# Attention in two-part float32 on one core: raw queries loaded once, their low part written to the other half, masks in three operations

## The reference

```python
scores = scale * np.matmul(q, k.transpose(0, 1, 3, 2))
rel = pos[:, None] - pos[None, :]
is_global = pos[None, :] < int(n_global)
is_local = (rel >= 0) & (rel < int(n_local))
keep = is_global | is_local
dist = np.where(is_global & ~is_local, float(n_local), np.abs(rel).astype(np.float32))
bias = -slopes[:, None, None] * dist[None, :, :]
scores = np.where(keep, scores + bias, -1000000000.0)
a = softmax(scores); out = a @ v
```

## Time and profile before

| what | value |
|---|---|
| median of 3 runs | 793.82 us (793.75 to 794.51) |
| profiled execution | 794.11 us; its span 792.4 us |
| busy time in the span | PE 740.9 us (94%), DVE 548.1 (69%), ACT 461.7 (58%), POOL 165.9 (21%) |
| attention | from the start to about 220 us |
| DMA | 151.65 MB, mean 191 GB/s |
| raw loads in attention | k_raw 64 x 208 KB, q_raw 64 x 192 KB |

### The profile page before, as it was taken

One profiled execution on the slowest core, in us unless ns is written; L12 is line 12 of the kernel. 1 busy time (PEld: TensorE's weight loads), 2 busy tenths in 40 slices (PEclk: granted clock), 3 DMA queues, 4 the chain that ended last, 5 costly groups with the idle time before them and its releaser, 6 DMA issues. The chain is left out here.

```text
span 792.4 us, 15792 instructions
## 1 busy us (share of the span) xinstructions
PE 740.9 (94%) x5585; PEld 662.7 (84%) x5588; DVE 548.1 (69%) x1499; ACT 461.7 (58%) x931; POOL 165.9 (21%) x189
## 2 busy tenths in 40 slices
PE   2899999999959999999999839999999999999997
PEld 2799999999938888898888627888888888889895
DVE  6878778777477979887777667767675758585420
ACT  3889899899535555565545315454636363636360
POOL 8100000000030232222321202142323232323221
PEclk9999999999969999999999959999999999999999
DMA  8999988986264676545763126676767676759751
GB/s 178 218 212 247 242 213 232 203 233 155 98 211 156 223 248 229 188 143 196 252 232 113 36 77 210 187 222 186 222 185 220 186 223 186 221 169 314 230 120 43
DMA packets 64106, 151.65 MB, mean 191 GB/s; under 512 B 12294, under 2 KB 15750, under 8 KB 64016
## 3 DMA queue, kind: packets, MB, share of 16 engines
q1 hardware_dynamic: 52512, 114.77, 49.2%
q0 software_dynamic: 11504, 35.72, 18.0%
HBM read 118.84 MB, written 16.67 MB: 171 GB/s over the span
## 5 line engine op out<-in xcount | busy, mean ns | idle before, releaser
L2006 PE MATMUL r_ph<-r_xh,r_w1h 128*128 128x384 f32 x256 | 90.7, 354 | 0.0
L2006 PE MATMUL r_ph<-r_xh,r_w1l 128*128 128x384 f32 x256 | 86.2, 337 | 0.0
L2006 PE MATMUL r_ph<-r_xl,r_w1h 128*128 128x384 f32 x256 | 85.8, 335 | 0.0
L604 ACT ACTIVATE pr<-pr,nmx 128x232 f32<-128x232 f32 (+1 forms) x192 | 79.9, 466 | 4.3 <-DVE nmx L710 2.9
L710 DVE CUSTOM_DVE_ANT_0 pr<-sc,bias 128x232 f32<-128x232 f32 (+1 forms) x192 | 65.0, 375 | 19.0 <-PE sc L478 17.7
L611 ACT ACTIVATE prt<-tp 128x384 f32<-128x384 f32 (+1 forms) x128 | 65.4, 536 | 20.4 <-PE tp L490 16.9
L2020 PE MATMUL r_py<-r_w2h,r_hh 128*128 128x512 f32 x192 | 76.3, 398 | 0.0
L2020 PE MATMUL r_py<-r_w2h,r_hl 128*128 128x512 f32 x192 | 75.1, 391 | 0.0
L2020 PE MATMUL r_py<-r_w2l,r_hh 128*128 128x512 f32 x192 | 74.9, 390 | 0.0
L518 PE MATMUL op<-vo,prt 128*128 128x128 f32 x384 | 69.5, 276 | 3.7 <-ACT prt L611 1.9
L477 PE MATMUL sc<-kk,qh 128*128 128x256 f32 x192 | 59.0, 328 | 14.7 <-POOL alive L439 14.3
(11 more groups left out here) (340 smaller groups left out, 1970.4 us busy)
## 6 DMA issues: line engine op xcount, KB each, us to landing
r_w<-moe_w SPq DMA_DIRECT2D x64, 512.0 KB, 5.7
m_w<-moe_w SPq DMA_DIRECT2D x36, 512.0 KB, 6.3
row_buf<-moe_w SPq DMA_DIRECT2D x9, 2048.0 KB, 8.4
r_w2l<-r_w POOLq DMA_DIRECT2D x32, 512.0 KB, 5.4
k_raw<-kI SPq DMA_DIRECT2D x64, 208.0 KB, 6.8
q_raw<-qT SPq DMA_DIRECT2D x64, 192.0 KB, 7.3
vo<-vL SPq DMA_DIRECT2D x16, 384.0 KB
x_rows<-row_buf SPq DMA_DIRECT2D x4, 1536.0 KB, 6.2
```

Of the source, the lines that this page charges most:

```text
L604: nc.scalar.activation(pr[n % PRS][:, t, lo:CW], pr[n % PRS][:, t, lo:CW], ACT.Exp, bias=nmx[n % PRS][:, t:t + 1], scale=-1.0).then_inc(ex ...
L2006: last = nc.tensor.matmul(ph[m % 4][:, 0:CAP], w[:, c, m * P:(m + 1) * P], x[:, c, :], start=(c == 0 and a == 0), stop=(c == KC - 1 and a ...
```

## The change

Raw queries are loaded once per head, into partitions 0 to 63; k is still loaded twice. `qq` holds q's high part in its upper half and q's low part in its lower half: DVE reads partitions 0 to 63 and writes 64 to 127. `kh` is k's high part in both halves, `kl` k's low part in partitions 0 to 63. The first product is qq with kh over 128 rows (high with high, low with high), the second qq's high half with kl over 64 rows. The zero memsets go.

The limits are loaded from ACT's queue, ahead of its first activation; SP starts with the raw loads, in the order pair 0, v of pair 0, pair 1, v of pair 1. POOL writes 768 into `rel` for keys after the query (one more link). DVE scales `rel` by 2^-40 before the limits arrive; masks are then three operations of full size (distances in units of 2^-40, capped by the limit for global keys, and whole numbers for masked keys), and a head's bias is one product per table. The third split now follows the first maxima, the fourth the second; the bias tables of heads 1 to 7 stand in steps 2, 5, 8, ... 20; the splits of pair 1 move by one step.

```diff
-def mask(link, rel, kpos, lims, isg, loc, keep, dist, shift=0.0, between=None):
+def mask(link, rel, kpos, lims, isg, loc, keep, dist, shift=0.0):
...
-            qh = [fb(f"qh{s}", [P, 2, S], F32R) for s in range(2)]
-            ql = [fb(f"ql{s}", [P, 2, S], F32R) for s in range(2)]
-            kk = [fb(f"kk{s}", [P, 2, KW], F32R) for s in range(2)]
+            qq = [fb(f"qq{s}", [P, 2, S], F32R) for s in range(2)]
+            kh = [fb(f"kh{s}", [P, 2, KW], F32R) for s in range(2)]
+            kl = [fb(f"kl{s}", [P, 2, KW], F32R) for s in range(2)]
...
                     for half in range(2):
-                        w = slice(half * D, half * D + D)
-                        sp.dma_start(k_raw[s][w, hh, :], kI[g, hh]).then_inc(raw_loaded[s][hh], 16)
-                        sp.dma_start(q_raw[s][w, hh, :], qT[g, hh * D:hh * D + D]).then_inc(raw_loaded[s][hh], 16)
+                        sp.dma_start(k_raw[s][half * D:half * D + D, hh, :], kI[g, hh]).then_inc(raw_loaded[s][hh], 16)
+                    sp.dma_start(q_raw[s][0:D, hh, :], qT[g, hh * D:hh * D + D]).then_inc(raw_loaded[s][hh], 16)
...
-                sp.dma_start(ints[:, 0:1], n_global.partition_broadcast(P)).then_inc(ints_loaded, 16)
-                sp.dma_start(ints[:, 1:2], n_local.partition_broadcast(P)).then_inc(ints_loaded, 16)
                 load_raw(0)
-                load_head(1, 0)
                 load_v(0)
-                load_head(1, 1)
+                load_raw(1)
                 load_v(1)
...
+                link(g.affine_select(out=rel[:, CA:].rearrange("p (t j) -> p t j", j=P), in_=rel[:, CA:].rearrange("p (t j) -> p t j", j=P),
+                                     compare_op=ALU.is_ge, fill=float(S), base=0, pattern=[[0, 2], [-1, P]], channel_multiplier=1))
                 assert link.n == RELS
-                link(g.memset(ql[0][D:P].bitcast(F32), 0.0))
...
-                link(g.memset(ql[1][D:P].bitcast(F32), 0.0))
...
-                        nc.tensor.matmul(to, qh[s][:, hh, q], kk[s][:, hh, keys], start=True, stop=False)
-                        last = nc.tensor.matmul(to, ql[s][:, hh, q], kk[s][:, hh, keys], start=False, stop=True)
+                        nc.tensor.matmul(to, qq[s][:, hh, q], kh[s][:, hh, keys], start=True, stop=False)
+                        last = nc.tensor.matmul(to, qq[s][0:D, hh, q], kl[s][0:D, hh, keys], start=False, stop=True)
...
-                    dst, src = (kk[s][:, hh, :], k_raw[s][:, hh, :]) if is_k else (qh[s][:, hh, :], q_raw[s][:, hh, :])
+                    dst, src = (kh[s][:, hh, :], k_raw[s][:, hh, :]) if is_k else (qq[s][0:D, hh, :], q_raw[s][0:D, hh, :])
...
+                act.dma_start(ints[:, 0:1], n_global.partition_broadcast(P)).then_inc(ints_loaded, 16)
+                act.dma_start(ints[:, 1:2], n_local.partition_broadcast(P)).then_inc(ints_loaded, 16)
                 act.wait_ge(filled, 1)
...
-                        g, c = n // 6 + 1, n % 6 - 1
+                        g, c = n // 6 + 1, n % 6 - (2 if n < 6 else 1)
...
-                dve.wait_ge(ints_loaded, 2 * 16)
                 dve.wait_ge(filled, RELS)
+                link(v.tensor_scalar(rel_units[:], rel[:], UNIT, None, ALU.mult))
+                dve.wait_ge(ints_loaded, 2 * 16)
...
-                        w = slice(D, P)
-                        ins = v.tensor_tensor(kk[s][w, hh, :], k_raw[s][w, hh, :], kk[s][w, hh, :].bitcast(F32), ALU.subtract)
+                        ins = v.tensor_tensor(kl[s][0:D, hh, :], k_raw[s][0:D, hh, :], kh[s][0:D, hh, :].bitcast(F32), ALU.subtract)
                     else:
-                        ins = v.tensor_tensor(ql[s][0:D, hh, :], q_raw[s][0:D, hh, :], qh[s][0:D, hh, :].bitcast(F32), ALU.subtract)
+                        ins = v.tensor_tensor(qq[s][D:P, hh, :], q_raw[s][0:D, hh, :], qq[s][0:D, hh, :].bitcast(F32), ALU.subtract)
...
-                        v.scalar_tensor_tensor(out=dst[:, h, :], in0=dist[:, w], scalar=-slope, in1=pen[:, w],
-                                               op0=ALU.mult, op1=ALU.add).then_inc(biased, 1)
+                        v.tensor_scalar(dst[:, h, :], dist[:, w], -slope / UNIT, None, ALU.mult).then_inc(biased, 1)
...
-                    mask(link, rel[:], kpos[:], lims, isg[:], loc[:], tmp[:], dist[:], between=first_parts)
-                    link(v.tensor_scalar(pen[:], tmp[:], 1.0, BIG, ALU.subtract, ALU.mult))
+                    link(v.tensor_scalar(local_units[:], lims[:, 1:2], UNIT, None, ALU.mult))
+                    link(v.tensor_scalar(outside[:], kpos[:], lims[:, 0:1], None, ALU.is_ge))
+                    link(v.scalar_tensor_tensor(out=far[:], in0=rel[:], scalar=lims[:, 1:2], in1=rel_units[:], op0=ALU.is_ge, op1=ALU.max))
+                    for c in (0, 1):
+                        split(0, c)
+                    link(v.scalar_tensor_tensor(out=dist[:], in0=outside[:], scalar=local_units[:], in1=far[:], op0=ALU.max, op1=ALU.min))
                     biases(0)
-                    dve.wait_ge(biased, 3)
-                    split(0, 2)
                     for n in range(STEPS):
                         if n < ALL_UNITS:
                             maxima(n)
-                        if n == 0:
-                            split(0, 3)
-                        if 1 <= n < H:
-                            biases(n)
+                        if n < 2:
+                            split(0, 2 + n)
+                        if n % 3 == 2 and n // 3 + 1 < H:
+                            biases(n // 3 + 1)
...
-                        g, c = n // 6 + 1, n % 6 - 2
+                        g, c = n // 6 + 1, n % 6 - (3 if n < 6 else 2)
                         if g < PAIRS and 0 <= c < PARTS:
                             split(g, c)
+                        elif n == 6:
+                            split(1, PARTS - 1)
```

More of the change, by code:

```diff
@@ L41 @@
 BIG = 8e9
+UNIT = 2.0 ** -40
 SCALE = D ** -0.5
@@ L102, in mask @@
     link(v.scalar_tensor_tensor(out=loc, in0=dist, scalar=lims[:, 1:2], in1=keep, op0=ALU.is_lt, op1=ALU.mult))
-    if between is not None:
-        between()
     link(v.tensor_tensor(dist, loc, dist, ALU.mult))
@@ L221, in build @@
             ints = tb("ints", [P, 2], I32)
-            rel, kpos, isg, loc, tmp, dist, pen = (tb(x, [P, CW + P]) for x in ("rel", "kpos", "isg", "loc", "tmp", "dist", "pen"))
+            rel, kpos, rel_units, far, outside, dist = (tb(x, [P, CW + P]) for x in ("rel", "kpos", "rel_units", "far", "outside", "dist"))
+            fits, local_units = tb("fits", [P, 1]), tb("local_units", [P, 1])
             bias, bias0 = tb("bias", [P, H, CW]), tb("bias0", [P, H, P])
@@ L270, in build @@
             TURNS = H * QT_N
-            PAIRS, PARTS, RAW_LOADS, V_LOADS, TABLE_LOADS = B * H // 2, 4, 4, 3, 5
+            PAIRS, PARTS, RAW_LOADS, V_LOADS, TABLE_LOADS = B * H // 2, 4, 3, 3, 5
             ALL_UNITS, HEADS = B * UNITS, B * H
             STEPS = ALL_UNITS + LAG + 7
-            RELS, FILLS = 9, 24
+            RELS, FILLS = 10, 23
             def norm_step(hd):
@@ L656, in _ @@
                 link = Chain(dve, chain)
+                dve.wait_ge(filled, RELS)
+                link(v.tensor_scalar(rel_units[:], rel[:], UNIT, None, ALU.mult))
                 dve.wait_ge(ints_loaded, 2 * 16)
-                dve.wait_ge(filled, RELS)
                 link(v.tensor_copy(lims[:], ints[:]))
-                link(v.tensor_scalar(isg[:, 0:1], lims[:, 0:1], float(FAST_GLOBAL), None, ALU.is_le))
-                link(v.scalar_tensor_tensor(out=isg[:, 0:1], in0=lims[:, 1:2], scalar=float(FAST_LOCAL), in1=isg[:, 0:1],
+                link(v.tensor_scalar(fits[:], lims[:, 0:1], float(FAST_GLOBAL), None, ALU.is_le))
+                link(v.scalar_tensor_tensor(out=fits[:], in0=lims[:, 1:2], scalar=float(FAST_LOCAL), in1=fits[:],
                                             op0=ALU.is_le, op1=ALU.mult))
-                link(v.scalar_tensor_tensor(out=banded[:], in0=lims[:, 1:2], scalar=1.0, in1=isg[:, 0:1],
+                link(v.scalar_tensor_tensor(out=banded[:], in0=lims[:, 1:2], scalar=1.0, in1=fits[:],
                                             op0=ALU.is_ge, op1=ALU.mult))
@@ L734, in fast @@
                     nlink = Chain(dve, nchain)
-                    def first_parts():
-                        for c in (0, 1):
-                            split(0, c)
-                    mask(link, rel[:], kpos[:], lims, isg[:], loc[:], tmp[:], dist[:], between=first_parts)
-                    link(v.tensor_scalar(pen[:], tmp[:], 1.0, BIG, ALU.subtract, ALU.mult))
+                    link(v.tensor_scalar(local_units[:], lims[:, 1:2], UNIT, None, ALU.mult))
[4 more added lines that the diff above has]
+                    link(v.scalar_tensor_tensor(out=dist[:], in0=outside[:], scalar=local_units[:], in1=far[:], op0=ALU.max, op1=ALU.min))
                     biases(0)
-                    dve.wait_ge(biased, 3)
-                    split(0, 2)
                     for n in range(STEPS):
```

## The result

The changed kernel takes 870.01 us in the median (four runs, 862.74 to 880.63) where the kernel before, run beside it, takes 793.79: a ratio of 1.0928 (95% interval 1.0832 to 1.1025). It is 76 us slower between the medians. The forecast was 790.8; the rival that PE pays for the half-height product had the right mechanism and, with 31 to 61 us, too low a price.

What follows compares the result with a forecast made beforehand. PE was taken to bound steady attention, so only an earlier start of unit 14 counts. A chain gain of 4.0 us less 1.0 for PE's later start gave 3.0: 790.8 us against the median 793.82; range 788.4 to 794.4.

Steps and rivals of the forecast that it cites:

- the rival that PE pays for the half-height product: Attention score products: PE empties at each of 384 changes between 128 and 64 rows, 31 to 61 us slower; chance 0.14.
- The step that failed: Both score products in attention: weights and columns stay 128 and 256, so no PE cost was counted.
- deciding point of 12 ns: Score products: cost per height change from which the slower case holds, (3.0 + 1.6) / 384.
- the bound: Score products: emptying costs up to 0.16 us a change, a record of 0.28 less the 0.12 to the next start.
- The row that I weighed against it: Steady attention: products using 104 rows stand in a pattern where PE has no gap, cited against a height cost.
- no measurable change: Start-up: late limits or a 9 us branch delay PE by 2.5 us, leaving 1.5 us gain or less; chance 0.22.
- PE's start, 1.0 us later in the sum: Start-up: limits on ACT's queue meet k's packets, so PE's first product moves from 14.33 to 15.3 us.
- its length: PE's start-up branch between code paths: taken as 7.3 us as before, at least 3.8, at most perhaps 9.
- The chain from the first product to unit 14: Start of attention: 24.14 us including 0.5 for hand-overs, against 28.11 before, a gain of 4.0 us.
- Unit 3: Start of attention: its scores start 4.34 us after PE's start, against 3.23 before, giving back 1.1 us.
- The unit times "1.0" and 1.70: Start of attention: unit 3 without products with v takes 1.0 us, somewhat over half of a whole unit's 1.70.
- eight units without gate work at a third of 5.09: Between unit 3 and unit 14: eight units at steady spacing take 13.6 us of PE.

Runs made afterwards that it cites:

- e2: The kernel before with its second score product over 64 rows, one line changed: 867.89 us, ratio 1.0901.
- e1: The changed kernel with its second score product over 128 rows again, the lower half of kl zeroed by a POOL memset: 794.37 us, ratio 0.9999.
- e3: The changed kernel with the two products of each unit's second tile swapped, so 192 height changes instead of 384: 829.95 us, ratio 1.0459.
- e5: e1 with the two limit loads first on SP's queue again and the kl memsets at the end of POOL's list: 792.23 us, ratio 0.9970.
- e8: The changed kernel with 18 unused products of the mask table given to PE ahead of its branch: 873.81 us, ratio 1.0979.
- e4: As e1, but with the second score product over 96 rows instead of 128: 794.92 us, ratio 1.0008.
- e9: e5 with q loaded twice and the loads in the old order: 792.85 us, ratio 0.9988.
- e10: e5 with masks, biases and the order of splits as before the change: 792.21 us, ratio 0.9978.
- e6: e5 with SP waiting for the path flag after the raw loads of pair 0: 791.59 us, ratio 0.9964.
- e7: The kernel before with SP waiting for the path flag after the raw loads of pair 0: 793.67 us, ratio 0.9994.
- e11: e6 with the third and fourth split of pair 0 ahead of the first maximum: 790.63 us, ratio 0.9954.

## Why the prediction was wrong

**The step that failed** is "The weights and columns of both score products stay 128 and 256, so I take nothing for PE." The number of rows changed, from 128 to 64, and the cost hangs on it: e2 makes the loss with that slice alone and e1 takes it back. The slower rival named it, its count of 384 changes is right (e3 halves it and halves the loss), and its deciding point of 12 ns was passed fifteen times over. Its price was mis-sized twice. A change costs 0.18 us, not 0.08 to 0.16: the bound took only the time that overlapping records could lose. The weight load, which no longer starts ahead of its product, is a likely remainder, but how the 0.18 us divides is not shown. And at the half clock, where the products stand 0.50 apart instead of the 0.21 of e5, it costs 0.3, and with the changes the clock stays there for longer (e8): units 0 to 14 took 38.3 us where e1's take 25.7, 12.6 us for 56 changes, 2.5 more than 56 x 0.18.

The chance of 0.14 was too small for what was known. The Trainium skill (TensorEngine Tiling (Array Packing), Key Properties) says that a change of tiling mode drains TensorE, and among its Available Configurations 64 rows are one of their own; the runs agree, at 0.18 us each. The row that I weighed against it, the 104-row products, is of another kind: e4 puts 96 rows with 128. A row can only speak against a rule if it shows the case that the rule is about.

**Right:** the branch starts at 7.7 us, as said; the limits are converted at 5.96 (5.9); the split that writes to other partitions takes 0.95, no more than before; the masks leave DVE ahead of PE; and neither ACT waits for q nor PE for v after 15 us. In e1 and e5 a pair of heads takes 12.18 us, where 12.27 was forecast as unchanged; over 13 pairs that is 1.2 us, which no experiment took apart (it is there with loads and with masks undone, e9 and e10).

**Without the failed step** the forecast would still have been wrong, and the rival "no measurable change" right: that is e1, 0.9999. PE's start, 1.0 us later in the sum, is 2.2 later in the changed kernel and 2.8 in e1. In e1 0.7 us of this is its own memset, behind which the limits are converted later (branch from 8.4 us). The start of the branch is as predicted in the changed kernel; its length is not: 8.6 us instead of 7.3. In all kernels with the limits on ACT's queue it is 8.4 to 8.7, with the limits first on SP's 7.3 to 7.8 (e10's trace lacks the record). Whether the bytes queued by SP set it is not tested: the waits of e6 and e7 held nothing back. The chain from the first product to unit 14 had 24.1 us, and e5 took 26.4. Unit 3 came 0.3 later than worked out, with the first maximum 1.4 us behind PE's first product instead of 1.25, and units 3 to 14 took 21.8 instead of 19.8. Two terms are at fault there. The unit times "1.0" and 1.70 were read at the full clock, and e5 was at the half level up to 23.5 us: its units 3 and 4 took 1.52 and 2.82. e1, with the same order of steps and the full clock from 20.3 us, took 0.82 and 1.65 for them and 21.05 for units 3 to 14, so the clock can be 0.7 of the 2.0 us. The other is "eight units without gate work at a third of 5.09": that spacing was read where no late tables competed and the splits had been made in time. In e1 unit 6, the first of pair 1, starts 2.9 us after unit 5, and PE waits for DVE's split, which had waited for ACT's:

```profile
27.18 0.39 PE L475 MATMUL sc<-kh,qq 128*128 128x256 f32 x1 [0.56 <-DVE qq L688]
```

**Left open:** why the branch is about a microsecond longer with the limits on ACT's queue, what sets its 7 to 8 us at all, what brings the clock down and up, and how much of the 0.18 us is the drain and how much the load of weights that no longer starts ahead.

## What to carry to other kernels

Between 128-row products do not slice a contraction down to 64 rows to save zeros: the product is no cheaper, and each change cost 0.18 us of PE. Pad with zeros to 128 rows, or to 96 (which cost nothing; heights between 64 and 96 were not run); where 64 are needed, put such products side by side. When an edit changes any dimension of an instruction on the engine that sets the time, count the edges between its forms and price each by a run of its own if no row has one. Look at the issue times when an experiment is meant to hold something back: the waits of e6 and e7 delayed SP by a quarter of a microsecond and by nothing. And do not read a full busy column as a full engine: the count of instructions in the stretch and the PEld column show what it does.

## What was not expected of the hardware

PE can stay at the half clock for 51 us while its records cover all the time (e8: 22.5 to 73.7 us), with a change of height at every score product.

Some of DVE's operations last until an instruction of POOL has ended, others beside it keep their time. While POOL's memset of `kl` ran (3.6 to 6.7 us in e1), DVE's tensor-by-constant operation took 1.71 us instead of 0.43 and a conversion of two numbers 1.08 instead of 0.17:

```profile
3.60 1.71 DVE L658 TENSOR_SCALAR rel_units<-rel 128x360 f32<-128x360 f32 x1 [3.60 <-POOL rel L407]
...
5.67 1.08 DVE L660 CAST lims<-ints 128x2 f32<-128x2 int32 x1 [0.36 <-DMA ints<-n_local]
```

```profile
3.62 3.10 POOL L411 MEMSET kl<- 64x1664 f32 x2
```

The conversion ends at 6.75 us, where the memsets end at 6.72. An iota of POOL (17.8 to 21.1 us in e5, 17.6 to 20.9 in e11) does the same to the bias products, 1.39 and 2.62 us a pair; they end at 21.3 and 21.1, each 0.2 us behind the iota. In e1, where that pair begins after the iota, it takes 0.41.

```profile
17.82 3.32 POOL L447 IOTA lane_grid<- 128x3072 bf16 x1
```

The two-tensor split at 18.33 in e5, in the middle of this iota, keeps its 0.95 us. The Trainium skill (GPSIMD Engine Reference, Key points) names contention with DVE instructions in a 2-port mode or with two SBUF inputs. The one-input operations agree, if they run in such a mode, which no trace here says. The two-input split does not, beside an iota that has no input, and the measurement decides.
